# Sliding-window attention in a two-layer MoE kernel: transposes, value products and scores of two groups in one block at every second step

## What is computed

```python
# 1. attention with a window of 64 positions
scores = q @ k.transpose(0, 1, 3, 2) / sqrt(64)
rel = pos[:, None] - pos[None, :]
scores = where((rel >= 0) & (rel < 64), scores, -1e9)
attn = exp(scores - max(scores)); attn /= attn.sum(-1, keepdims=True) + 1e-9
x = (attn @ v).transpose(0, 2, 1, 3).reshape(2304, 512)
# 2. x = ((x @ w1) * (x @ w2)) @ w3 @ w_out
# 3. routing: each row goes to the one expert with the largest logit of x @ w_gate
#    y = relu(x @ e_w1[e]) @ e_w2[e], scaled by the softmax weight and sigmoid(x @ w_output_gate)[e]
```

## Time and profile before

| what | value |
|---|---|
| runs | 724.66 us (723.98 to 725.04) |
| the profiled execution | 726.28 us, of which the span between first and last instruction 724.5 us |
| PE busy | 709.9 us (98%) |
| DVE, ACT, GpSimd busy | 329.7, 298.6, 119.7 us |
| transposes of attention (L527) | 144 |
| rows of the scores (L515) and of the values (L537) | 576 and 576 |
| end of the weight phase: first scores of chunk 0 | 85.23 us |

### The profile page before, as it was taken

One profiled execution on the slowest core, in us unless ns is written; L12 is line 12 of the kernel. 1 busy time (PEld: TensorE's weight loads), 2 busy tenths in 40 slices (PEclk: granted clock), 3 DMA queues, 4 the chain that ended last, 5 costly groups with the idle time before them and its releaser, 6 DMA issues.

```text
span 724.5 us, 15149 instructions
## 1 busy us (share of the span) xinstructions
PE 709.9 (98%) x5139; PEld 646.8 (89%) x5140; DVE 329.7 (46%) x667; ACT 298.6 (41%) x721; POOL 119.7 (17%) x191
## 2 busy tenths in 40 slices
PE   5999999999999999999999999999999999999997
PEld 5889999999999999999999999888888888888885
DVE  3478554512234534542221648845356544562211
ACT  4367545422135444453211244444355544552121
POOL 5011111110011111111000000212222222222211
PEclk9999999999999999999999999999999999999999
DMA  9586212320012231202501014657265763511110
GB/s 288 193 300 224 68 30 73 104 88 1 1 55 70 66 110 60 78 25 79 198 1 44 1 48 157 237 187 220 80 222 183 240 192 111 203 34 43 32 43 30
DMA packets 48064, 80.14 MB, mean 111 GB/s; under 512 B 5326, under 2 KB 29902, under 8 KB 48017
## 3 DMA queue, kind: packets, MB, share of 16 engines
q1 hardware_dynamic: 42976, 64.01, 27.6%
q0 software_dynamic: 5040, 15.47, 6.2%
HBM read 70.03 MB, written 10.49 MB: 111 GB/s over the span
## 4 chain that ended last, share of the span: by engine, by line
PE 96%; DMA 2%; DVE 1%; ACT 1%; POOL 0%; issue 0%; POOLq 0%; SPq 0%; ACTq 0%
PE bank L461 28%; PE bank L463 27%; PE bank L462 27%; PE bank L537 3%; PE bank L671 3%; PE bank L515 2%; PE bank L527 2%; PE bank L649 1%; DMA wo<-in_w_out 1%; DMA w3r<-in_w3T 1%; PE bank L473 1%; PE bank L631 1%; PE bank L501 0%; PE bank L497 0%; PE bank L495 0%; POOL prob L1296 0%
## 5 line engine op out<-in xcount | busy, mean ns | idle before, releaser
L461 PE MATMUL bank<-Wh,abh 128*128 128x272 f32 (+1 forms) x288 | 84.3, 293 | 0.0
L463 PE MATMUL bank<-Wh,abl 128*128 128x272 f32 (+1 forms) x288 | 82.0, 285 | 0.0
L462 PE MATMUL bank<-Wl,abh 128*128 128x272 f32 (+1 forms) x288 | 81.8, 284 | 0.0
L732 ACT ACTIVATE prob<-prob,nmx 128x128 f32<-128x128 f32 x144 | 56.3, 392 | 60.2 <-DVE nmx L913 60.2
L996 DVE TENSOR_TENSOR wbuf<-raw,wbuf 128x1024 f32 (+1 forms) x64 | 75.3, 1221 | 11.9 <-ACT wbuf L797 11.8
L1296 POOL TENSOR_TENSOR prob<-prob,rec 128x384 f32<-128x384 f32 x48 | 39.8, 829 | 212.8 <-DVE rec L923 209.7
L1178 DVE TENSOR_TENSOR hTl<-bank,hTh 128x512 fp32r<-128x512 f32 x44 | 28.4, 685 | 95.6 <-ACT hTh L835 95.6
L461 PE MATMUL bank<-wbuf,hTh 128*128 (+1 forms) x176 | 70.7, 402 | 0.0
L461 PE MATMUL bank<-wbuf,xsTh 128*128 (+1 forms) x176 | 70.4, 400 | 0.0
L463 PE MATMUL bank<-wbuf,hTl 128*128 (+1 forms) x176 | 68.8, 391 | 0.0
L463 PE MATMUL bank<-wbuf,xsTl 128*128 (+1 forms) x176 | 68.6, 390 | 0.0
(11 more groups left out here) (199 smaller groups left out, 1498.2 us busy)
## 6 DMA issues: line engine op xcount, KB each, us to landing
raw<-in_expert_w SPq DMA_DIRECT2D x64, 512.0 KB, 4.6
qT<-in_qT SPq DMA_DIRECT2D x24, 192.0 KB, 2.9
kT<-in_kT SPq DMA_DIRECT2D x24, 192.0 KB, 3.3
x_rows<-x_sb POOLq DMA_DIRECT2D x18, 256.0 KB, 2.3
w3r<-in_w3T SPq DMA_DIRECT2D x8, 512.0 KB, 4.1
wo<-in_w_out SPq DMA_DIRECT2D x8, 256.0 KB, 7.1
woT<-in_w_outT SPq DMA_DIRECT2D x4, 512.0 KB, 7.8
vA<-in_v SPq DMA_DIRECT2D x16, 128.0 KB, 2.1
```

The costliest lines, as they stand in the source:

```text
L461: pe.matmul(dst, lh, rh, start=first, stop=False)
L462: pe.matmul(dst, lh, rl, start=False, stop=False)
L463: return pe.matmul(dst, ll, rh, start=False, stop=last)
L732: ex_i = act.activation(prob[k % 4][:, cols], prob[k % 4][:, cols], ACT.Exp, bias=nmx[:, row], accum_out=sums[:, row])
```

## The change

The unit of attention becomes the pair of groups (both heads of one third): six pairs per batch, `NP`. The work is asked for by step with four small functions, and everything of a pair stands in one place. `fold_scored` and `fold_weighed` translate for the weight phase.

```diff
-        score_bank = lambda h: bank[4 + 3 * h]
+        unit_of = lambda p: divmod(p, NGRP)
+        score_bank = lambda h: bank[5 + 2 * h]
+        turn_bank = lambda h: bank[5 - h]
+        buf_of = lambda p, h: p % 2 * 2 + h
...
+        def scored(e):
+            return e // 2 + 1 if e % 2 == 0 and e // 2 + 1 < NP else None
+        def turned(e):
+            return e // 2 - 1 if e % 2 == 0 and e >= 2 else None
+        def valued(e):
+            return e // 2 - 2 if e % 2 == 0 and e >= 4 else None
+        def weighed(e):
+            return 0 if e == 0 else (e + 1) // 2 if e % 2 and (e + 1) // 2 < NP else None
...
+        def fold_scored(i):
+            return i - 2 if i in (2, 3) else scored(i - 2) if i > 3 else None
```

On PE, the block behind a step:

```diff
+            def score(b, p):
+                G = b * NP + p
+                u, j = unit_of(p)
+                copied = G if p == 0 else G - 1
+                pe.wait_ge(qk_in[j], (b * (PAIRS // 2) + u + 1) * (16 * 2))
+                if copied > 0:
+                    pe.wait_ge(pt_ok, 2 * copied - 1)
+                if G > 0:
+                    pe.wait_ge(masked, 2 * G)
...
+            def turn(b, p):
+                G = b * NP + p
+                pe.wait_ge(masked, 2 * min(G + 2, (b + 1) * NP))
+                if G > 0:
+                    pe.wait_ge(pt_ok, 2 * G)
+                for h in range(2):
+                    pe.wait_ge(p_ok, 2 * G + h + 1)
                     for i in range(3):
-                        mm = pe.transpose(bank[5][:, i * P:(i + 1) * P], prob[(k - 1) % 4][:, i * P:(i + 1) * P], ident[:, :])
+                        mm = pe.transpose(turn_bank(h)[:, i * P:(i + 1) * P], prob[buf_of(p, h)][:, i * P:(i + 1) * P], ident[:, :])
                     mm.then_inc(pt_done, 1)
...
+            def attend(b, e, s):
+                if turned(e) is not None:
+                    turn(b, turned(e))
+                if valued(e) is not None:
+                    value(b, valued(e))
+                if s is not None:
+                    score(b, s)
```

`value(b, p)` waits for the pair's `pT` copies and the last pair's `o_lo`, then does twelve products into bank 6. There are four `pT` buffers now (the room is taken from an unused one). ACT and DVE follow: `exps` does six exponentials in a row, `turn_out` copies one head's transposes, `value_hi` and `value_lo` take 384 columns at once. ACT's order in the weight phase, behind the copy of W's high part:

```diff
+                own()
+                if i >= 2 and turned(i - 2) is not None:
+                    turn_out(0, turned(i - 2), 0)
+                    turn_out(0, turned(i - 2), 1)
+                if i >= 2 and valued(i - 2) is not None:
+                    value_hi(0, valued(i - 2), 0)
...
                 if n == 1 and it + 3 < KF:
                     hi_w3(it + 3)
+                if fold_scored(i) is not None:
+                    exps(0, fold_scored(i))
                 if i in w12_steps:
                     hi_w12(w12_steps.index(i))
```

In a hidden tile `turn_out` of head 0 stands between the copy of a and that of the product. The gate columns' 16-wide products (`G1_product`) move from bank 5 to bank 4. The loads:

```diff
             load_qk(0, 0)
+            load_qk(0, 1)
+            load_qk(0, 2)
+            load_w3(3)
             load_v(0, 0)
-            load_qk(0, 1)
             load_w12(0)
+            load_w3(4)
+            next_qk(1, 0)
             load_v(0, 1)
-            load_w3(3)
-            load_qk(0, 2)
-            load_w3(4)
-            load_v(0, 2)
             load_w12(1)
-            next_qk(1, 0)
             load_w3(5)
-            load_w12(2)
-            next_v(1, 0)
             next_qk(1, 1)
             next_qk(1, 2)
+            load_w12(2)
+            load_v(0, 2)
             load_w12(3)
+            next_v(1, 0)
             load_w3(6)
+            load_w12(4)
             next_v(1, 1)
-            load_w12(4)
             load_w12(5)
             load_w3(7)
...
             with sp.Fori(2, UNITS // 2) as u:
-                next_qk(u, 0)
-                next_v(u, 0)
-                next_qk(u, 1)
-                next_qk(u, 2)
-                next_v(u, 1)
-                next_v(u, 2)
+                for j in range(NGRP):
+                    next_qk(u, j)
+                for j in range(NGRP):
+                    next_v(u, j)
```

More of the change, by code:

```diff
@@ L270, in for_chunks, with pair_x @@
                 chunk(cc, c, batches, b, 1 if c == 0 else 0, final)
[L273 to L286, removed]
+        def pair_x(t, p, parity):
+            u, j = unit_of(p)
+            c = parity * S + j * 3 * WIN
+            return t[:, :].rearrange("p (k c) -> p k c", c=SUPER)[:, 2 * u:2 * u + 2, c:c + 3 * WIN]
+        pair_o = lambda t: t[:, 0:6 * WIN].rearrange("p (h c) -> p h c", c=3 * WIN)
         row_tiles = [(n, tt, i * CT + tt) for i, n in enumerate((1, 0)) for tt in range(CT)]
@@ L502, in W_half @@
                 mm.then_inc(W_done, 1)
[L505 to L516, removed]
-                                               kT[rows, r * S + key_start(i):r * S + key_start(i) + P], start=True, stop=True)
-                            if i % 3 == 2:
-                                mm.then_inc(s_done, 1)
@@ L800, in chunk @@
             def chunk(cc, c, batches, b, parity, final):
+                turns = lambda e: b is not None and turned(e) is not None
                 def hidden_tile(f):
@@ L821, in chunk @@
                 for n, tt, i in row_tiles:
-                    around(attend, attend_end, b, KF + i, parity, lambda: row_tile(i, n, tt))
+                    if b is not None and KF + i == NSTEP - 1:
+                        value_hi(b, LAST, parity)
+                    row_tile(i, n, tt)
+                    if turns(KF + i):
+                        turn_out(b, turned(KF + i), 0)
+                    attend(KF + i)
             def xs_out(s, src=bank[0]):
@@ L916, in weigh, with masks @@
[L916 to L929 removed]
+            def masks(b, p):
+                for h in range(2):
+                    g, pr = 2 * (b * NP + p) + h, prob[buf_of(p, h)]
+                    dve.wait_ge(s_done, g + 1)
+                    dve.scalar_tensor_tensor(pr[:, :], score_bank(h)[:, 0:3 * P], SEQ_SCALE,
+                                             mask[:, 0:3 * P] if unit_of(p)[1] == 0 else mask[:, P:4 * P],
+                                             ALU.mult, ALU.add).then_inc(masked, 1)
+                    dve.wait_ge(masked, g + 1)
+                    dve.tensor_reduce(nmx[:, stat(p, h)], pr[:, :].rearrange("p (i c) -> p i c", c=P),
+                                      AX.X, ALU.max, negate=True).then_inc(nmx_ok, 1)
@@ L984, in own @@
                         for j in range(0, KF, 2):
-                            g = wo_lo_out(j, DM, WXC, bank[5][:, j * LG:(j + 2) * LG].rearrange("p (j c) -> p j c", c=LG))
+                            g = wo_lo_out(j, DM, WXC, bank[4][:, j * LG:(j + 2) * LG].rearrange("p (j c) -> p j c", c=LG))
                         g.then_inc(g1_lo, 1)
-                fold_step(attend, attend_end, i, own)
-                if i == 2:
-                    weigh(0, 0)
+                if i == len(w_order) - 1:
+                    value_lo(0, LAST, 0)
+                own()
+                if fold_scored(i) is not None:
+                    masks(0, fold_scored(i))
+                if i >= 2 and valued(i - 2) is not None:
+                    value_lo(0, valued(i - 2), 0)
             weight_splits(len(w_order) - 1)
@@ L999, in chunk, with weights, attend @@
             def chunk(cc, c, batches, b, parity, final):
+                def weights(e):
+                    if b is not None and weighed(e) is not None:
+                        weigh(b, weighed(e))
+                def attend(e):
+                    if b is not None and scored(e) is not None:
+                        masks(b, scored(e))
+                    if b is not None and valued(e) is not None:
+                        value_lo(b, valued(e), parity)
                 def hidden_tile(f):
-                    weigh(b, f)
+                    weights(f)
                     fc = slice(f * CH, (f + 1) * CH)
@@ L1031, in chunk @@
                             xs_out(0, bank[7])
-                    around(attend, attend_end, b, KF + i, parity, lambda: row_tile(i, n, tt))
+                    if b is not None and KF + i == NSTEP - 1:
+                        value_lo(b, LAST, parity)
+                    row_tile(i, n, tt)
+                    attend(KF + i)
             def xs_out(s, src=bank[0]):
@@ L1311, in chunk @@
                 if b is not None:
-                    for k in range(NG):
-                        attend(b, k, parity)
+                    normalise(b)
                 if final:
```

189 lines of the change are left out of this document (101 added, 88 removed).

## The result

| what | before | after |
|---|---|---|
| runs, median | 724.66 us | 727.91 us (726.58 to 728.61) |
| the profiled execution | 726.28 us, span 724.5 | 728.52 us, span 726.7 |
| ratio of the medians, 95% interval | | 1.0043 (1.0029 to 1.0058) |
| first scores of the weight phase | 27.16 us | 25.56 us |
| end of the weight phase: first scores of chunk 0 | 85.23 us | 91.88 us |

The changed kernel is slower by 0.43%, where 0.2% can be told from no change. The forecast was 723.3. The time is outside the range given (721.0 to 727.2), above it.

The account below looks back on a forecast made before the run. TensorE, busy 709.9 of 724.5 us, was taken to bound the kernel. Terms -7.55 - 1.27 + 0.96 + 3.0 + 3.2 + 0.35 gave -1.31 us, so 723.3 us from a median of 724.66, range 721.0 to 727.2.

Parts of the forecast that it names:

- The switches: TensorE's big matmuls are interrupted 9 times per batch instead of 14, saving 1.89 us per batch, 7.55 us for four.
- rival 4: A switch costs by length, not by block, so joined blocks save about half: 727.1 us, chance 0.07.
- The waits for GpSimd: In the weight phase, two waits of the transposes for normalised probabilities disappear, saving 1.27 us.
- The third block of later batches: Without value products as cover, scores wait 0.32 us for ScalarE's copy from shared bank 5; 0.96 us for three batches.
- The wait of 3.0: Weight phase, after half 4 (24 big matmuls): pair 2's scores wait 3.0 us for ScalarE's copy behind a w3 split and exponentials.
- Rival 3: Three late w3 pieces, 5.65 us each, make blocks after halves 6, 8, 10 wait 6.2 us more: 729.5 us, chance 0.13.
- halves 6, 8 and 10: Weight-phase blocks after these runs of 24 big matmuls wait for ScalarE's copies behind w3 splits, 3.2 us in all.
- rival 5: The clock falls in the 3.0 us wait, so the next halves run at 1.2 GHz: 726.4 to 729.5 us, chance 0.04.
- The handover: End of the weight phase: a longer copy and subtraction of the last values delay the first chunk by 0.35 us.

Follow-up runs that it names:

- experiment 8: The changed kernel with 100 unused semaphore increments at the start of TensorE's stream: 733.25 us against 724.65 for the kernel before.
- the 716.3 us: The changed kernel with later w3 splits, first-pair head 0 transposes in bank 6, and the last w1 split earlier on VectorE: 716.32 us against 724.65.
- experiment 1: The changed kernel with SP's weight-phase loads in the order of the kernel before: 730.4 us against 725.1 for the kernel before.
- experiment 6: The changed kernel with head 0's transposes of the first pair in bank 6: 723.46 us against 724.65 for the kernel before.
- experiment 2: The changed kernel with pair 1's six exponentials ahead of the split of w3 piece 3 on ScalarE: 724.09 us against 725.1 for the kernel before.
- experiments 8 and 9: The first has its own line; the second is the kernel before, unchanged, profiled again: 724.09 us, w3 piece 3 loading in 3.43 us.

## Why the prediction was wrong

Its own steps, in its order.

- **The switches (-7.55): right.** A chunk with attention is 1.44, 1.46 and 1.41 us shorter. Two waits are in that, 0.37 before the scores of the third block (forecast 0.32) and 0.09 before the last values (not forecast: the joined block waits for the previous pair's low part). Put back, they make 1.90 per batch, forecast 1.89. With that rival 4 (a switch costs by length, so that half is saved) is out. In the first batch the 1.89 isn't measured: it is what the other terms leave over. The rows of a block bear it out: twelve value products lie between 117.47 and 118.31, 0.84, where 0.85 was worked out.

```profile
116.83 0.71 PE L538 MATMUL bank<-ident,prob 128*128 128x128 f32 x5
117.47 0.45 PE L551 MATMUL bank<-pT,vA 128*64 128x64 f32 x8
...
118.31 0.89 PE L524 MATMUL bank<-kT,qT 64*64 64x128 f32 x24
```

- **The waits for GpSimd (-1.27): right.**
- **The third block of later batches (+0.96): right**, 1.11 measured, 0.37 in each of three.

```profile
106.35 0.82 PE L538 MATMUL bank<-ident,prob 128*128 128x128 f32 x6
107.47 0.40 PE L524 MATMUL bank<-kT,qT 64*64 64x128 f32 x5 [0.30 <-issue]
```

- **The wait of 3.0: right in its mechanism, mis-sized.** It measured 5.49. All of the difference is one term, the load of piece 3. The forecast let the split start at 35.39, as in the one execution of before, 3.48 behind the issue; in the changed kernel it started 5.96 behind it. The row of 5.65 stood beside it and was used only as a bound for the pieces behind it. That is the step that failed: one row of a load was taken for its duration in another program, and no range was given to the 3.0. Rival 3 had the right mechanism, for the wrong pieces: those behind halves 6, 8 and 10 came in time (their splits start 3.28, 3.50 and 3.36 behind the issue), and their blocks wait 2.83 in all, forecast 3.2.
- **The clock (rival 5, chance 0.04): wrong.** It fell, and it cost 2.63. The argument against it was that PE stood idle for 7.7 us ahead of its first matmul and the page shows the upper level in that slice. That row was misread. In the changed kernel the trace's first record of the clock begins at 12.31, in the kernel before at 14.48, and the page shows the upper level wherever it has no record. PE's own rows show the lower level behind the idle start. In the kernel before, matmuls of 256 columns follow one another after 0.21 us from 8.01 to 13.43, where 0.12 is the pace at the upper level:

```profile
8.01 0.41 PE L462 MATMUL bank<-wol,w3h 128*128 128x256 f32 x1
8.22 0.41 PE L463 MATMUL bank<-xTh,w3l 128*128 128x256 f32 x1
8.43 0.41 PE L461 MATMUL bank<-xTh,w3h 128*128 128x256 f32 x1
```

In the changed kernel the pace goes from 0.21 to 0.12 at 12.27, where the record begins. So "no row shows the lower level" was wrong: the trace of before had the price of a slow half, some 0.09 us on each of its 24 matmuls or 2.2 us, and a stretch of idle time with the lower level behind it, though it can't tell that a wait in mid-work does the same. The Trainium skill, TensorE: Matmul & The Clock Gate, the part on avoiding throughput drops, says that idle gaps between bursts bring the clock down; the runs agree in five of the six kernels whose longest wait before scores was over 2 us (5.49, 4.89, 3.27, 2.85 and 2.6), and not in the sixth (3.01). The misread row was the only ground for putting this term at nothing in the sum, which is the second step that failed, and 0.04 was far too little.
- **The handover (+0.35)** measured 0.30.

Two numbers beside the sum were worked out wrong, and neither moves the forecast. Without the waits for the copy the sum would have been -8.5 and not -7.5 (-1.31 less 0.96, 3.0 and 3.2); and three pieces of 5.65 for 3.48 are 6.5 us more and not 6.2, so that rival 3 stood for 729.8.

With 5.49 for 3.0 and 2.63 for the clock the sum would have been +3.8, that is 728.5; the median is 727.9. Of the +5.1 that the forecast lacked, half is the load and half is the clock that fell in the wait. With a load of 3.45 and the clock up (experiment 8, less its late start) the same program is at 723.5 to 724.1, near the forecast of 723.3: that was the time of a kernel whose piece 3 lands as it did in before.

## What to carry to other kernels

When an engine copies something that TensorE waits for, no work that waits for a load may stand ahead of that copy in its queue: moving the splits of five weight pieces one step back was worth some 9 us here, more than all the saved switches. A wait that rests on one load's duration has the slowest such row for an upper end, and a wait of some us in TensorE's stream is priced with the lower clock level behind it. Whether the clock is up is read from the distance between matmuls of one size as well, since the clock row of the page shows the upper level where the trace has no record. And when a saving in the steady part is paid for in one stretch of the start, that stretch can be mended by itself, as the 716.3 us show.

## What the runs showed of the hardware that was not expected

- **The clock.** In the profiled executions it fell in or behind waits of 5.49, 4.89, 3.27, 2.85, 2.6 and 2.06 us and stayed for 3.41 or 6.83 us at the lower level; it did not fall after one of 3.01, nor after any of 1.9 or less. The length of the wait alone doesn't tell: 2.06 fell (experiment 1, its second stretch), 3.01 didn't. Nor does the fall come at a fixed place: it came 1.50 us before PE went on (experiment 1, 38.62 against 40.12) and 0.85 us after (experiment 6, 47.65 against 46.80). In experiment 2 the same program took 723.1 to 724.4 in some runs and 725.5 to 726.0 in others.
- **Instruction packets.** The 512 KB load of piece 3 took 3.4 to 3.5 us in the three profiled kernels without a 16 KB instruction packet well inside it and 4.9 to 6.0 in the nine with one. That the packet is the cause is likely, not shown, and it holds for this load alone (experiments 8 and 9). The change moved the packet against the load, from 35.52 behind a landing at 35.37 to 32.55 inside one from 30.45 to 36.39, and the load came 2.5 us late.
- **Semaphore increments on TensorE's queue** took 0.15 us each: a hundred took 15.3 us, of which 6.6 lay in PE's first wait, and moved the first product by 8.8 us.
- **The start.** PE's first products, behind 7.7 us without work, ran at half pace: 0.21 us for 256 columns up to 12.27 in the changed kernel, 0.12 from there on.
